# A linear-attention, feed-forward and expert kernel on one core: half of the gate products and the last logits taken out of the stretch between two blocks

## What is computed

```python
# attention: a decaying state per head (4 x 8 heads, 768 steps, 48 wide)
y[t] = r[t] @ (state + (u * k[t]) v[t]^T);  state = w * state + k[t] v[t]^T
# x: 3072 tokens x 384
h = x @ w_in;  x2 = (h - tanh(h)) @ w_out                     # 2048 wide
xn = x2 / (norm(x2) + 1e-6);  en = emb / (norm(emb) + 1e-6)
logits = xn @ en.T / tau;  expert = argmax(logits, 1)         # 8 experts
gate = softmax(logits)[expert]
out = gate * (relu(x2 @ w1[expert]) @ w2[expert])             # 1024 wide
```

## Time and profile before

| | us |
|---|---|
| median of 3 runs | 910.67 (909.86 to 911.35) |
| the profiled execution | 908.92 |
| its span, first to last instruction | 907.1 |
| PE busy | 849.6 (94%) |
| DVE, ACT, POOL busy | 599.7, 474.3, 331.7 |
| mean granted clock of PE | 0.975 of full speed |

### The profile page before, as it was taken

One profiled execution on the slowest core, in us unless ns is written; L12 is line 12 of the kernel. 1 busy time (PEld: TensorE's weight loads), 2 busy tenths in 40 slices (PEclk: granted clock), 3 DMA queues, 4 the chain that ended last, 5 costly groups with the idle time before them and its releaser, 6 DMA issues. The chain is left out here.

```text
span 907.1 us, 18422 instructions
## 1 busy us (share of the span) xinstructions
PE 849.6 (94%) x5028; PEld 758.1 (84%) x5029; DVE 599.7 (66%) x962; ACT 474.3 (52%) x1213; POOL 331.7 (37%) x373
## 2 busy tenths in 40 slices
PE   4888888999999999999999999699999999999995
PEld 3677776788899899899899898589899898998994
DVE  9889995899999999999999998611112112112120
ACT  3344445666777777777777766323333323333331
POOL 8577774222243343343343323022222322222211
PEclk8799999999999999999999999879999999999998
DMA  8698994311586786786886798378856846711100
GB/s 229 193 266 257 264 257 129 95 44 52 196 280 217 269 279 218 268 277 220 268 276 220 241 313 270 124 253 330 320 187 222 305 160 222 292 36 38 48 2 1
DMA packets 109177, 184.59 MB, mean 203 GB/s; under 512 B 11371, under 2 KB 35085, under 8 KB 109136
## 3 DMA queue, kind: packets, MB, share of 16 engines
q1 hardware_dynamic: 95184, 168.54, 57.0%
q0 software_dynamic: 3968, 10.82, 3.5%
q10 hardware_dynamic: 9984, 4.72, 1.9%
HBM read 119.55 MB, written 65.86 MB: 204 GB/s over the span
## 5 line engine op out<-in xcount | busy, mean ns | idle before, releaser
L1070 POOL TENSOR_TENSOR ew_l<-ew_raw,ew_h 128x512 fp32r<-128x512 f32 x96 | 126.8, 1328 | 213.1 <-DVE poly L1264 213.1
L987 PE MATMUL y_ps<-wout_h,g_h 128*128 128x392 f32 x384 | 132.0, 344 | 4.0 <-ACT x_sb L1178 3.0
L988 PE MATMUL y_ps<-wout_l,g_h 128*128 128x392 f32 x384 | 130.7, 340 | 0.0
L989 PE MATMUL y_ps<-wout_h,g_l 128*128 128x392 f32 x384 | 130.5, 340 | 0.0
L1419 DVE TENSOR_TENSOR ex_hT_l<-e_bank,ex_hT_h 128x512 fp32r<-128x512 f32 x62 | 39.9, 686 | 125.3 <-ACT ex_hT_h L1592 125.3
L987 PE MATMUL h_ps<-xT_h,win 128*128 (+1 forms) x288 | 113.1, 393 | 1.7 <-DVE diff L1245 1.6
L988 PE MATMUL h_ps<-xT_l,win 128*128 (+1 forms) x288 | 112.7, 391 | 0.0
L989 PE MATMUL h_ps<-xT_h,win 128*128 (+1 forms) x288 | 112.4, 390 | 0.0
L1462 POOL DMA_INDIRECT out_dram<-ex_o_sb,put_i x31 | 31.1, 1002 | 205.8 <-ACT ex_o_sb L1576 205.8
L1158 ACT ACTIVATE g_h<-poly 128x512 fp32r<-128x512 f32 x96 | 61.1, 636 | 84.8 <-DVE poly L1264 84.3
L1592 ACT ACTIVATE ex_hT_h<-e_bank 128x512 fp32r<-128x512 f32 x62 | 33.7, 597 | 120.2 <-PE e_bank L1497 116.1
(11 more groups left out here) (193 smaller groups left out, 1969.0 us busy)
## 6 DMA issues: line engine op xcount, KB each, us to landing
ew_raw<-in_w SPq DMA_DIRECT2D x96, 256.0 KB, 3.2
w_h<-ew_h SPq DMA_DIRECT2D x96, 256.0 KB, 3.3
w_l<-ew_l SPq DMA_DIRECT2D x96, 256.0 KB, 2.5
w_ex<-w_h SPq DMA_DIRECT2D x14, 1536.0 KB, 7.2
w_ex<-w_l SPq DMA_DIRECT2D x14, 1536.0 KB, 11.5
rT_sb<-in_rT SPq DMA_DIRECT2D x48, 96.0 KB, 3.2
kT_sb<-in_kT SPq DMA_DIRECT2D x48, 96.0 KB, 3.4
k_sb<-in_k SPq DMA_DIRECT2D x24, 192.0 KB, 3.4
```

What stands on the lines that cost most here:

```text
L987: pe.matmul(out, lh, rh, start=start, stop=False)
L988: pe.matmul(out, lh, rl, start=False, stop=False)
L989: return pe.matmul(out, ll, rh, start=False, stop=stop)
L1070: pool.tensor_tensor(ew_l[:, slot, :], raw, ew_h[:, slot, :].bitcast(F32), ALU.subtract).then_inc(ew_l_made, 1)
```

## The change

Three edits, and a bank that carries one of them.

1. **Last low piece.** In the last step of the last group POOL waits for the last low part of g (`gl_done`), where it waited for `g_done`.
2. **Last logits.** After the last group ACT copies the 8 logit columns of each of the four banks from PSUM into `logits`, in four instructions, and only then makes the four 392-column copies to `x2_sb`. The 32-column copy from `x2_sb` is gone there.
3. **Gates.** `place_gates` stands at the end of `route_vector`, ahead of the block's barrier. `route_tensor` gets `keep_warm` 10, a wait for the first two of the four placed parts, the first 12 gate products, and `keep_warm` 3. In the experts' block PE starts with the transposes; its `keep_warm` 4 is gone.
4. **Bank.** `bank7` is allocated once, ahead of all other banks, for all blocks: as attention's eighth bank, as `usq[1]`, and as the bank in which the gate sums stay across the barrier.

```diff
+        bank7 = whole.enter_context(nc.psum_tensor("bank7", [P, 512], F32))
...
-        usq = [psum(f"usq{i}", [P, G]) for i in range(2)]
+        usq = [psum("usq0", [P, G]), bank7]
...
             last.then_inc(ids_turned, 1)
+            keep_warm(pe, h_ps[1], ident, 10)
+            pe.wait_ge(gates_placed, 2)
+            turn_gates(pe, 0)
+            keep_warm(pe, h_ps[1], ident, 3)
+
+        def turn_gates(pe, first):
+            for n in range(first, first + PART):
+                last = pe.matmul(gate_ps, oh_slot[:, n, :], rhs_gate[:, n, :, :].rearrange("p a s -> p (a s)"),
+                                 start=(n == 0), stop=(n == NT - 1))
+            return last
...
             step(dve.tensor_tensor(gate_l[:, :], gates[:, 1, :], gate_h[:, :].bitcast(F32), ALU.subtract))
+            for at in range(0, NT, PART):
+                for part, x in ((0, gate_h[:, at:at + PART].bitcast(F32)), (1, gate_l[:, at:at + PART])):
+                    dve.tensor_tensor(rhs_gate[:, at:at + PART, part, :], in_tile[:, at:at + PART, :],
+                                      wide(x, COLS), ALU.mult).then_inc(gates_placed, 1)
...
-                        if not is_first(g):
+                        if last and f == KF - 1:
+                            pool.wait_ge(gl_done, KF * CH)
+                        elif not is_first(g):
                             wait_apart(pool, passed_pool, (g_done, KF * g + f + 1))
...
                 for b in range(B):
+                    act.wait_ge(y_done, B * (CH - 1) + b + 1)
+                    kept = act.activation(logits[:, B * (CH - 1) + b, :], y_ps[b][:, DM:DL], ACT.Copy)
+                kept.then_inc(logits_kept, 1)
+                for b in range(B):
                     finish(CH - 1, b)
-                keep_logits(CH - 1)
...
-                place_gates()
                 x_low(0, 0, 0)
                 take_gates()
...
                 pe.sem_inc(tile_done, 1)
-                keep_warm(pe, y_ps[1], ident, 4)
-                turn_gates(0)
                 transpose_tokens(0, 0, 0)
-                turn_gates(PART).then_inc(gates_turned, 1)
+                turn_gates(pe, NT // 2).then_inc(gates_turned, 1)
```

More of the change, by code:

```diff
@@ L131, in build @@
             attention(nc, rT, kT, r, k, v, w, u_row, w_in, w_outT, emb, tau, x_dram, load_group, xt_sb, xt_stored,
-                      ident, consts, rtau, win_h, win_l, w_logit)
-            placed = feed_forward(nc, x2_dram, xg_sb, load_group, xg_loaded, xt_stored, ident, consts, win, w_ex, w_out, w_logit,
+                      ident, consts, rtau, bank7, win_h, win_l, w_logit)
+            turn_gates = feed_forward(nc, x2_dram, xg_sb, load_group, xg_loaded, xt_stored, ident, consts, bank7, win, w_ex, w_out, w_logit,
                          sumsq, w12, w12_h, w12_l, rows_sb, get_row, put_row, expert_at, ends_at, gathered,
                          first_loaded)
-        experts(nc, x2_dram, out, w_ex, w12_h, w12_l, ident, rows_sb, get_row, put_row, gate, expert_at, ends_at, gathered,
-                first_loaded, *placed)
+        experts(nc, x2_dram, out, w_ex, w12_h, w12_l, ident, bank7, rows_sb, get_row, put_row, gate, expert_at, ends_at, gathered,
+                first_loaded, turn_gates)
 def attention(nc, rT, kT, r, k, v, w, u_row, w_in, w_outT, emb, tau, x_dram, load_group, x_sb, x_stored,
-              ident, consts, rtau, win_h, win_l, w_logit):
+              ident, consts, rtau, bank7, win_h, win_l, w_logit):
     EP = 32
@@ L190, in attention @@
         mask = sb("mask", [P, 4 * P])
-        banks = [psum(f"bank{i}", [P, 512]) for i in range(8)]
+        banks = [psum(f"bank{i}", [P, 512]) for i in range(7)] + [bank7]
         scores = [[banks[0], banks[1]], [banks[2], banks[3]]]
@@ L678, in _, with feed_forward @@
                 keep_warm(pe, banks[1], ident, 4)
[L681 removed]
+def feed_forward(nc, x2_dram, x_sb, load_group, x_loaded, x_stored, ident, consts, bank7, win, w, w_out, w_logit,
                  sumsq, w12, w12_h, w12_l, rows_sb, get_row, put_row, expert_at, ends_at, gathered,
@@ L809, in feed_forward @@
         id_ps = h_ps[0][:, 0:COLS]
+        gate_ps = bank7[:, 0:2 * COLS]
         GROUP = 8
+        PART = NT // 2
         r_dve = sem("r_dve")
@@ L1285, in _, with experts @@
                 route_vector(dve)
-    return in_tile, oh_slot, rhs_gate, gate_h, gate_l
-def experts(nc, x2_dram, out, w, w12_h, w12_l, ident, rows_sb, get_row, put_row, gate, expert_at, ends_at, gathered,
-            first_loaded, in_tile, oh_slot, rhs_gate, gate_h, gate_l):
+    return turn_gates
+def experts(nc, x2_dram, out, w, w12_h, w12_l, ident, bank7, rows_sb, get_row, put_row, gate, expert_at, ends_at, gathered,
+            first_loaded, turn_gates):
     with ExitStack() as ctx:
@@ L1306, in experts @@
         sb("w_room", [P, SLOTS, HALVES, PARTS * WIDE], F32R)
-        banks = [psum(f"e_bank{i}", [P, 512]) for i in range(8)]
+        banks = [psum(f"e_bank{i}", [P, 512]) for i in range(7)]
         w_loaded = [[sem(f"w_loaded{slot}_{part}") for part in range(PARTS)] for slot in range(SLOTS)]
@@ L1343, in experts @@
         t_ps = banks[6]
-        gate_ps = banks[7][:, 0:2 * COLS]
+        gate_ps = bank7[:, 0:2 * COLS]
         gate_high = sb("gate_high", [P, ST])
-        PART = NT // 2
         get_ready = sem("get_ready")
@@ L1420, in tile @@
                                           ALU.subtract).then_inc(hT_split, 1)
[L1422 to L1427, removed]
                 def take_gates():
```

2 lines of the change are left out of this document (1 added, 1 removed).

## The result

The changed kernel took **901.42 us** in the median of four executions (900.43 to 906.03; a fifth, which is not in that median, took 903.13); the kernel before took 910.68 beside it (909.86 to 911.35). The ratio is 0.991, with a 95% interval of 0.9881 to 0.994. Six more executions on another chip gave 903.38 (900.17 to 904.57) beside 910.70, a ratio of 0.9916 (0.9895 to 0.9937). The forecast was 902.4, in a range of 900.4 to 906.2.

A forecast was written before the change was run, and what follows sets the result against it. PE was busy 94%; time could be won around the barrier ahead of the experts, where it waited and ran at half clock. 5.96 + 2.36 = 8.3 us gave 902.4 us, range 900.4 to 906.2.

The forecast's parts named there:

- The last low piece: Feed-forward's end: with POOL's piece behind it, DVE's last `g_l` is shorter and PE's last product starts 0.64 us earlier.
- the last logits: After the feed-forward's last bank: one narrow copy follows it instead of 0.76 us of copies, saving 0.53 us.
- shift: Routing starts and the first fetch is issued 1.17 us earlier.
- The gates ahead of the barrier: Placements and gate products run before the barrier; PE arrives last, and transposes start at 588.5 instead of 593.34, 4.8 us earlier.
- LDWEIGHTS: Gate products: trace rows, 0.111 us each at full and 0.213 at half clock, kept over the skill's clock-independent rule.
- Behind the barrier: Transposes to first product take 2.0 us, not 3.12; first product 5.96 us earlier, another 2.4 if the clock holds.
- I think it holds: PE's clock stays full around the barrier through the first tile, winning 2.4 us on its first twelve products.
- rival 1: The clock falls near the barrier all the same: gain 4.8 us, 905.9, or 2.9 if already during list products; chance 0.20.
- The drains: At the barrier: POOL's drain ends 1.17 us earlier, at 587.35; PE is last, 0.8 us after POOL.
- Rival 2: The fetch lands later and POOL's drain holds the barrier; with 2 us more, 903.6 or 907.1; chance 0.06.
- Rival 4: Moved PSUM banks slow all 96 feed-forward steps; 0.087 us a step eats the 8.3 us gain; chance 0.03.
- Downstream: Experts' later weight loads also come earlier; the fourth tile needs them at 616 instead of 624, and they are covered.

The follow-up runs named there:

- e_pool: The kernel before with only the last low piece's edit (POOL waits for `gl_done`): 909.48 us, ratio 0.9993 to before.
- e_logits: The kernel before with only the last logits' edit (narrow copies ahead of the wide ones): 909.89 us, ratio 0.9993 to before.
- e_no10: The changed kernel without `keep_warm` 10 between list products and gate products: 906.95 us, ratio 0.9958 to before.
- e_mix: The changed kernel plus two unused 128-column products behind each group of list products but the last: 904.0 us, ratio 0.993 to before.
- e_gates: The changed kernel with the low-piece and logits edits taken back, so gates and bank alone: 903.11 us, ratio 0.9929 to before.
- e_no3: The changed kernel without `keep_warm` 3 behind the gate products: 903.73 us, ratio 0.9922 to before.
- e_again2: A second execution of the changed kernel without `keep_warm` 3 behind the gate products: 902.33 us.
- e_best: The changed kernel without `keep_warm` 3, plus two unused 128-column products behind the first and second list groups: 903.72 us, ratio 0.9934 to before.
- e_warm: The kernel before plus `keep_warm` 13 on PE behind the list products, nothing moved: 906.72 us, ratio 0.9952 to before.

## Why the prediction was right, point by point

**The last low piece and the last logits: right.** Forecast -0.64 and -0.53, measured 0.62 and 0.58 (e_pool, e_logits), together 1.21 against a shift of 1.17. The narrow copy took 0.18, less than its nearest row (0.23). Of the two explanations for the long `g_l`, the overlap with POOL's piece is shown, since moving that piece alone brought it to 0.69. POOL's piece waited 4.33 us and nobody waited for it.

**The gates ahead of the barrier: right in place, one term too long.** Gates started at 25.73 from the mark (forecast 25.74), PE's drain was last by 0.72 over POOL's (0.75), and the pause at the barrier was 0.45 (0.42). Twelve gate products took 1.53 in records, starts to the next loop 1.36 (1.33). `keep_warm` 10 took 2.74, not 3.6. I had priced it by the 0.36 a turn of `keep_warm` 16; here a turn took 0.27 at the same clock, and no run shows why. The 0.9 us became a pause (0.70), since PE waits for DVE there. At full clock that cost nothing.

**LDWEIGHTS: the rows decide.** e_no10 shows twelve gate products in 2.77 us at half clock, and e_mix the same twelve in 1.53 at full. The Trainium skill, "TensorE: Matmul & The Clock Gate", section "LDWEIGHTS (loading the stationary operand)", makes a load of weights last the number of its columns over 1.2, in ns, without a word of the clock: an estimate of 0.107 us each, 1.3 for twelve. That fits only the second, and I had kept the rows.

**Behind the barrier: right where the clock held.** Transposes to first product took 1.94 in the changed kernel and 1.95 in e_mix (forecast 2.0), where it was 3.12 before. With the twelve products of the first tile at full clock the second tile came 8.23 earlier than before (e_mix; forecast 8.3). Of this 7.97 were left at the end of the span.

**"I think it holds": too sure.** This is the step that failed. The clock fell in both profiled executions of the changed kernel, at 584.8 and 582.3, and in e_gates, e_no3 and e_again2 too, each time among the 32-column products or just behind them. The prediction had named the reason against itself, that the fall at 584.41 came after narrow products, and gave it 0.20. What it got wrong in that rival is the length: 3.4 to 6.8 us instead of the 17.1 of before, and here the ten turns decide, since without them it was 17.1 again (e_no10). So the clock was back before the transposes, and the 3.5 us that rival 1 took off behind the barrier were not lost. The fall cost time only ahead of the barrier: `keep_warm` 10 took 4.61 at half clock, and PE reached its gate products at 590.79, 0.93 after the second part was placed (589.86) and 1.17 later from the mark than in e_mix. The second tile came at 38.26 and 38.06 against 36.74: 1.5 and 1.3 us. The gain behind the mark was 6.6 and 6.8 us; the forecast's 8.3 was right for a clock that holds, 8.0 in e_mix.

**The drains: as forecast.** POOL's took 3.6 us in every kernel, whenever it began. In the changed kernel the fetch was issued at 588.08 and landed 3.3 us later, which is when the drain ended (591.4). Rival 2 had no case: PE was last in every version that kept the three turns.

**The banks: no price.** Rival 4 needed 0.087 us a step. From its first square to its last the feed-forward took 400.2 to 400.4 us in all twelve profiled executions, eight with the new allocation and four with the old, so a place of the banks costs no more than 0.003 us a step. The squares into `bank7` in the changed kernel, against rows 14 (those into `usq[0]` have a median of 577):

```profile
L1166 ACT ACTIVATE bank<-h_ps x48: 576/582/618, 165.7 to 563.9; 128x512 f32<-128x512 f32 x48
```

Attention uses `bank7` too. The first square, which follows it, started at 161.15 on the mean of the eight and at 161.32 on the mean of the four; single executions scatter by 4.6 us there, so this shows no price and can't rule out some tenths of a us.

**Downstream: covered, with less to spare.** In the experts PE waited for no weights, in the fourth to sixth tile or later. But the loads hardly came earlier, while the tiles came 6.7 us earlier. The third fetch was issued at 31.73 from the mark (30.90 before), since the barrier opens later than before. The second expert's first load came at 36.09 (36.61), the first half of its weights had landed at 47.5 and the second at 57.5 (57.0). The fourth tile, their first user, took the first half at 57.45 (64.15 before), and the second some 14 us later. So about 10 us are left where there were about 15; a further gain ahead of the barrier would use these up first.

**Why the median still fell by more than 6.6.** The profiled executions scatter by 4.5 us in the start of the last square alone (559.37 to 563.89), and all of that comes from attention, since the feed-forward took the same in each. The falls of the clock in attention differ from one execution to the next too, but they don't account for it: e_no10 and e_best spent 23.9 us each at half clock ahead of the mark, and their marks are 3.1 us apart. Before's profiled execution, with 560.06, is 1.56 ahead of the mean of the four with the old allocation (561.62); that would account for most of the 1.75 us by which it lay under the median, which the prediction had left unexplained. Scatter of that size is enough for the first measurement (-9.3 us) and the second (-7.3) to differ, and the two ratios agree within their intervals. The forecast of 902.4 took the clock to hold, and in neither profiled execution did it. The 6.6 and 6.8 us of the traces would put the median near 904, inside the range. That 902.4 lies between the two medians, 901.42 and 903.38, is partly luck: what the clock took back, 1.3 to 1.5 us, is no more than the scatter.

**Left open.** What moves the end of attention by up to 4.6 us from one execution to the next isn't known, nor what makes the clock fall there in some executions and not in others. Nor is it settled whether the three turns behind the gates earn their 0.67 us by keeping the first tile at full clock: seven traces agree with it, and the times can't tell.

## What to carry to other kernels

When a trace has a stretch at half clock, ask for two prices, that of the work and that of the clock: here filling the wait bought about 3.6 us by the times, and moving twelve small products about 1.7 by an estimate from the traces. An experiment that takes one part away still holds all the others: e_no10's 2.9 us look like the move alone until the 1.2 us of the small edits are taken off. Before comparing two traces, choose a mark just ahead of the edit and measure from it; from the span's start this change looks like 2.8 us, from the mark it is 6.6. An edit worth half a microsecond can be shown by such distances where its time can't show it. It can be lost again at the next thing on the path, here a clock that falls, and behind the clock's return the distances themselves move by 0.8 us.

## What the hardware showed that I had not expected

- PE's records can be nearly without a gap and the clock still falls. In the changed kernel PE was busy 1.89 of 2 us and 1.93 of 2 us in the windows around the fall at 584.8, with products of 32 columns. With 128-column products between the same groups it held both times (e_mix, e_best).
- Where wide products followed it, a fall lasted 3.4 or 6.8 us (eight falls near the barrier: two in the changed kernel's two profiled executions, four in the two without the three turns, one each in e_gates and e_best); with the wait left empty it lasted 17.1 us (before, e_logits, e_no10) or 20.5 (e_pool). e_warm doesn't fit: 3.4 and then 10.2.
- POOL's drain behind an indirect DMA took 3592 to 3661 ns in the four kernels whose rows stand here or in rows 6, wherever the fetch stood, and in the changed kernel it ended when the fetch landed. At the barrier ahead of the feed-forward, with no indirect DMA before it, the same drain took 389 ns in the kernel before. So the fetch can hold a barrier through the drain of the engine that issued it.
- DVE's placement that overlaps the issue of POOL's indirect DMA by 0.40 us took 0.56, and the last one, clear of it, 0.55, while `g_l`, which overlapped a POOL subtraction by 0.77, took 1.32 instead of 0.69. The changed kernel's timeline:

```profile
588.08 1.16 POOL L833 DMA_INDIRECT rows_sb<-x_dram,get_row  x1 [16.07 <-DVE get_row L941]
...
588.84 0.56 DVE L954 TENSOR_TENSOR xT_l<-tanh,xT_l 128x384 fp32r<-128x384 f32 x1
...
590.25 0.55 DVE L954 TENSOR_TENSOR xT_l<-tanh,quad 128x384 fp32r<-128x384 f32 x1
```
